# Another order of preparation for the first block of a fused attention and feed-forward kernel, with its feature sums on GpSimd

## The chip, the cores and the metric

The kernel runs on one NeuronCore of a Trainium2 chip. Five engines work side by side, each through its own instruction queue in order: TensorE (PE in the profile; its weight loads are PEld), VectorE (DVE), ScalarE (ACT), GpSimd (POOL) and SyncE (SP), which here issues all the DMAs. They wait for one another through semaphores. The metric is the device time of one execution in microseconds.

## What is computed

Attention over 4 batches, 8 heads, 576 positions and 64 features a head, and then two gated feed-forward layers over the 2304 tokens:

```python
# two attentions per head, added
q_d, k_d, v_d = (mean of 4 neighbouring positions)       # 144 positions
out_up = repeat(softmax(q_d k_d^T / 8) v_d, 4)
out_local = softmax(where(|i - j| < 4, q k^T / 8, -1e9)) v
x = (out_up + out_local) as (2304 tokens, 512)
x = silu(x @ moe_w_in) @ moe_w_out                        # 512 -> 2048 -> 512
h = x @ moe2_w_in
out = (h * sigmoid(1.702 h)) @ moe2_w_out
```

## The kernel before

**The attention part** goes through 16 units; a unit is two heads of one batch (`Unit`, number `n`). In a unit, PE makes the banded scores (`band_scores`, L1088 and L1095), then transposes the probabilities of the unit before (`group`, L1077), makes the scores of the averaged positions (`avg_scores`, L1118), and multiplies the unit before with its values (`band_product` L1147, `avg_product` L1158). DVE reduces and subtracts the maxima (L1017, L1020, L1024), sums the rows (L1030), takes the reciprocal (L1034), sums four neighbouring positions of the next unit's q and k (`sums`, L1005), and writes the unit before into `x` (L1050). ACT takes the exponentials (L944, L956), normalises (L975) and copies out of PSUM (L928, L932, L964). GpSimd sums v (L887, L895), normalises the band (L890) and makes two of the first layer's weight sums (`sum_weights`, L905 to L911). All engines run `iterations`: unit 0, units 1 to 15, and a last step 16 that only finishes unit 15.

**The feed-forward part** (`Ffn`) goes over 6 blocks of 768 tokens: 3 of the first layer, 3 of the second. It multiplies in a scheme with seven products instead of eight for a 2 by 2 division into quarters, and each factor is split into a rounded part and a rest (`xs`, `wh`, `gr`; index 0 is the rounded part, index 1 the rest), so that a product is three matmuls a tile. In `first` PE makes 8 pairs of 42 matmuls into `hid` (L309), in the order of the table `FIRST`; in `second` seven stages of 48 matmuls into `yp` (L332), in the order of `SECOND`. What the products need of a block's features are seven quarters and their sums: B11, B21, B22 as they are, T1, T3, T2, T4 as differences, made in place (`sum_x`, L256). Each is rounded by ACT (`round_x`, L241) and its rest made by DVE (`rest_x`, L245), in the order of `FILLS`.

**The order around the change** is written out by hand. For the first block this preparation is strewn into the attention units by `early`: ACT rounds the weights of batches 0 to 2 in units 3 to 5 and the features in units 6 and 8 to 13; DVE makes weight rests in units 4 to 6, feature rests in 7, 9 to 12, 14, 15 and the four sums in 8, 9, 10 and 13. ACT's `early` of unit `n` from 8 waits for `x_done` of all units up to `n-1`, and stands ahead of its normalising (L975). For the later blocks `prepare_x` does it in the stages of `second`. SP starts with the loads of q and k of two units, and issues the writing back of the first weight sums (`store_first`) only when all 16 units are written, since it stands in `ffn.sync`. PE begins with 11 matmuls on an identity (`WARM`, L1186), whose results nobody uses.

## Time and profile before

| | |
|---|---|
| median of 3 runs | 831.03 us (829.6 to 832.05) |
| profiled execution | 829.3 us, of which its span 827.4 us |
| PE busy, share of the span | 804.7 us, 97% |
| DVE / ACT / POOL busy | 655.6 / 536.1 / 176.1 us |
| attention: from the start to the first feed-forward matmul | 0 to 117.2 us |
| feed-forward: from there to the end | 117.2 to 827.4 us |

In a line of the timeline stand the start in us from the span's beginning, the time taken, the engine, the line of the code, the operation, the tile written and those read, the shapes, how many instructions are merged (x...), and in brackets how long the engine had been idle just before and what ended that. The start of one instruction and the end of the one before it on the same engine overlap by up to 0.1 us, so costs on a path are taken from start to start. A busy PE of 97% says that there is little idle time, not that the matmuls run at their fastest: 4032 of them are the feed-forward part.

### The profile page before, as it was taken

What the parts mean: (1) busy time and instruction counts of PE and PEld (TensorE: products, weight loads), DVE (VectorE), ACT (ScalarE), POOL (GpSimd) and SP (SyncE); (2) the same over time, 40 slices, a digit from 0 to 9 for tenths busy, and PEclk for the clock granted to TensorE, in tenths of its full rate; (3) what the DMA queues carried; (4) which work ended last, traced back from release to release, by engine and by line L of the source; (5) the groups of instructions that cost most, each with busy time, mean ns of one, the idle gap of its engine ahead of it and who ended that gap; (6) DMA issues with size and microseconds to landing.
All of it is one profiled execution on the core that took longest, in us unless ns stands there. A gap on an engine that the chain in (4) does not pass through costs nothing.

```text
span 827.4 us, 15637 instructions
## 1 busy us (share of the span) xinstructions
PE 804.7 (97%) x5787; PEld 776.3 (94%) x5787; DVE 655.6 (79%) x945; ACT 536.1 (65%) x864; POOL 176.1 (21%) x191
## 2 busy tenths in 40 slices
PE   7998999999999999999999999999999999999998
PEld 4776679999989999999999999999999999999997
DVE  6999959889998967798867888899756677665465
ACT  4887765567745577745578565687455777465763
POOL 6766656702025511025300000000000000000000
PEclk9999999999999999999999999999999999999999
DMA  7877748757677897768886787876987878877773
GB/s 216 241 224 208 223 147 292 255 202 258 206 259 245 270 321 257 258 203 273 263 298 237 229 264 251 268 248 229 307 270 259 268 254 265 285 255 271 256 271 125
DMA packets 98315, 205.42 MB, mean 248 GB/s; under 512 B 8416, under 2 KB 56032, under 8 KB 98240
## 3 DMA queue, kind: packets, MB, share of 16 engines
q1 hardware_dynamic: 98240, 204.42, 75.0%
q8 instruction: 47, 0.77, 0.4%
q14 instruction: 28, 0.23, 0.1%
HBM read 160.87 MB, written 43.52 MB: 247 GB/s over the span
## 4 chain that ended last, share of the span: by engine, by line
PE 79%; DVE 13%; issue 4%; ACT 2%; POOL 1%; DMA 1%; DVEq 0%; SPq 0%; POOLq 0%; ACTq 0%
PE hid L309 40%; PE yp L332 35%; DVE gr L482 2%; DVE wh L284 2%; DVE smb L1030 1%; DVE xs L245 1%; DVE x L1050 1%; PE pt L1077 1%; DVE sums L1005 1%; DVE mxb L1017 1%; DVE pband L1020 1%; PE po L1147 1%; DMA sums_in<-G 1%; ACT yt L928 1%; PE sc L1095 1%
## 5 line engine op out<-in xcount | busy, mean ns | idle before, releaser
L309 PE MATMUL hid<-xs,wh 128*128 128x384 f32 x2016 | 352.4, 334 | 3.1 <-DVE hw L462 1.8
L309 PEld LDWEIGHTS hid<-xs,wh 128*128 128x128 f32 x2016 | 349.2, 188 | 5.5 <-issue 5.2
L332 PE MATMUL yp<-gr,wh 128*128 128x384 f32 x2016 | 350.9, 334 | 1.7 <-DVE gr L482 1.7
L332 PEld LDWEIGHTS yp<-gr,wh 128*128 128x128 f32 x2016 | 349.4, 188 | 2.3 <-issue 2.3
L275 ACT ACTIVATE wh<-wr 128x1024 fp32r<-128x1024 f32 (+1 forms) x164 | 164.5, 1003 | 156.1 <-PE hid L309 122.4
L482 DVE TENSOR_TENSOR gr<-G,gr 128x768 fp32r<-128x768 f32 x144 | 138.5, 971 | 48.3 <-ACT gr L382 48.3
L382 ACT ACTIVATE gr<-G 128x768 fp32r<-128x768 f32 x144 | 121.8, 846 | 68.9 <-PE yp L332 67.6
L284 DVE TENSOR_TENSOR wh<-wr,wh 128x1024 fp32r<-128x1024 f32 x76 | 89.7, 1181 | 21.5 <-ACT wh L275 21.5
L349 ACT ACTIVATE G<-G 128x1152 f32<-128x1152 f32 x48 | 55.8, 1161 | 0.0
L457 DVE TENSOR_TENSOR hv<-p,hid 128x384 f32<-128x384 f32 x48 | 26.4, 549 | 28.4 <-PE hid L309 19.3
L472 DVE TENSOR_TENSOR G<-hv,hid 128x384 f32<-128x384 f32 x48 | 26.5, 552 | 26.5 <-PE hid L309 25.9
L245 DVE TENSOR_TENSOR xs<-x,xs 128x768 fp32r<-128x768 f32 x42 | 41.2, 981 | 5.6 <-ACT xs L241 5.6
L241 ACT ACTIVATE xs<-x 128x768 fp32r<-128x768 f32 x42 | 34.9, 832 | 10.0 <-DVE x L1050 10.0
L424 DVE TENSOR_TENSOR G<-G 128x384 f32<-128x384 f32 x48 | 29.1, 607 | 8.4 <-ACT G L349 8.4
L469 DVE TENSOR_TENSOR G<-hw,hid 128x384 f32<-128x384 f32 x48 | 26.3, 548 | 3.4 <-DMA sums_in<-G 2.3
L431 DVE TENSOR_TENSOR G<-G 128x384 f32<-128x384 f32 x48 | 28.4, 592 | 0.2
L549 POOL TENSOR_TENSOR G<-G 128x256 f32<-128x256 f32 x8 | 6.4, 806 | 103.0 <-DMA G<-in_w_in 54.5
L275 ACT ACTIVATE wh<-G 128x1024 fp32r<-128x1024 f32 (+1 forms) x16 | 15.3, 956 | 19.1 <-PE hid L309 19.1
L549 POOL TENSOR_TENSOR wt<-wt 128x256 f32<-128x256 f32 x12 | 10.4, 867 | 80.9 <-DMA wt<-in_w_out 45.9
L474 DVE TENSOR_TENSOR gr<-G,gr 128x384 fp32r<-128x384 f32 x48 | 27.4, 571 | 0.0
L462 DVE TENSOR_TENSOR hw<-hv,hid 128x384 f32<-128x384 f32 x48 | 26.3, 548 | 1.4 <-PE hid L309 0.9
L364 ACT ACTIVATE G<-hid 128x384 f32<-128x384 f32 x48 | 23.6, 492 | 5.7 <-PE hid L309 1.1
(90 smaller groups left out, 766.1 us busy)
## 6 DMA issues: line engine op xcount, KB each, us to landing
wh<-rests SPq DMA_DIRECT2D x72, 512.0 KB, 3.9
wr<-sums_out SPq DMA_DIRECT2D x48, 512.0 KB, 4.8
wr<-in_w_out SPq DMA_DIRECT2D x36, 512.0 KB, 5.2
rests<-wh SPq DMA_DIRECT2D x36, 512.0 KB, 3.4
wr<-sums_in SPq DMA_DIRECT2D x40, 384.0 KB, 4.1
wr<-in_w_in SPq DMA_DIRECT2D x40, 256.0 KB, 3.5
qk<-in_qkT SPq DMA_DIRECT2D x16, 576.0 KB, 5.4
G<-in_w_in SPq DMA_DIRECT2D x12, 512.0 KB, 6.2
```

The lines of the kernel that those rows point to most:

```text
L241: eng.activation(xs[:, 0, q], features(n, q), ACT.Copy).then_inc(self.x_hi, 1)
L245: eng.tensor_tensor(xs[:, 1, q], features(n, q), xs[:, 0, q].bitcast(F32), ALU.subtract).then_inc(self.x_lo, 1)
L275: eng.activation(wh[:, w % SLOTS, 0, 0:entries(w), :], raw(w), ACT.Copy).then_inc(w_hi, 1)
L284: eng.tensor_tensor(wh[:, w % SLOTS, 1, 0:e, :], raw(w), wh[:, w % SLOTS, 0, 0:e, :].bitcast(F32), ALU.subtract).then_inc(w_lo, 1)
L309: last = eng.matmul(hid[:, at, 0:HALF], lhsT=wh[:, w % SLOTS, part, a % 4, cc * P:(cc + 1) * P], rhs=xs[:, rest, q, cc, :], start=start an ...
L332: last = eng.matmul(yp[:, at + m, 0:HALF], lhsT=wh[:, w % SLOTS, part, p % 4, m * P:(m + 1) * P], rhs=gr[:, p, rest, :], start=start and p ...
L349: eng.activation(G[:, s % PAIRS, G12:G22 + 1, :], G[:, s % PAIRS, G12:G22 + 1, :], ACT.Silu, scale=scale).then_inc(self.gate, 1)
L382: eng.activation(gr[:, 2 * a:2 * a + 2, 0, :], G[:, 2 * a:2 * a + 2, at, :], ACT.Copy).then_inc(self.g_hi, 1)
L424: eng.tensor_tensor(G[:, p, G11, :], G[:, p, G12, :], G[:, p, G11, :], ALU.subtract).then_inc(self.t_sum, 1)
L431: eng.tensor_tensor(G[:, p, G12, :], G[:, p, G22, :], G[:, p, G12, :], ALU.subtract).then_inc(self.t_sum, 1)
L474: eng.tensor_tensor(gr[:, p, 1, :], G[:, p, G11, :], gr[:, p, 0, :].bitcast(F32), ALU.subtract).then_inc(self.b11_lo, 1)
L482: eng.tensor_tensor(gr[:, 2 * a:2 * a + 2, 1, :], G[:, 2 * a:2 * a + 2, SECOND[i][1], :], gr[:, 2 * a:2 * a + 2, 0, :].bitcast(F32), ALU.s ...
```

## The change

- `WARM` goes from 11 to 7.
- q and k get three buffers instead of two (the third is the place of `ffn.wt`), and the sums of four positions two buffers; three units are loaded at the start, and `sums` runs two units ahead: twice ahead of unit 0, and not in unit 14.
- `FILLS` has another order. `ROUNDED_W`, `ROUNDED` and `SUMMED` say in which units the first block is prepared: ACT rounds weights in 4, 6, 7 and features in 3, 5, 9, 10, 11, 13, 15; DVE makes the rests one unit later; the four sums are made by GpSimd, each in two halves of 128x384, in units 7 to 14, behind its weight sums. The wait for `x_done` is for one unit less.
- In the later blocks DVE makes each of the four sums behind another rest.
- PE makes the first three products of the first pair (18 matmuls) in step 16, ahead of the transposes of unit 15.
- ACT applies Silu to a small tile that is no longer needed, behind the normalising of unit 15.
- `store_first` for pairs 0 and 1 stands in the attention part, behind unit 15's loads.

```diff
-FILLS = (B11, T1, T3, T2, B21, B22, T4)
+FILLS = (B11, B21, T1, B22, T3, T2, T4)
...
-        def sum_x(eng, n, q):
+        def sum_x(eng, n, q, chunk=None):
...
-            eng.tensor_tensor(features(n, q), a, b, ALU.subtract).then_inc(self.x_sum, 1)
+            if chunk is None:
+                eng.tensor_tensor(features(n, q), a, b, ALU.subtract).then_inc(self.x_sum, 1)
+            else:
+                eng.tensor_tensor(features(n, q)[:, chunk], a[:, chunk], b[:, chunk], ALU.subtract).then_inc(
+                    self.x_sum if chunk else self.x_half, 1)
+                if not chunk:
+                    eng.wait_ge(self.x_half, XSUM[q])
...
-            for q in {B11: (T1, T3), T1: (T2,), B21: (T4,)}.get(FILLS[i], ()):
+            for q in {B11: (T1,), B21: (T3,), T1: (T2,), B22: (T4,)}.get(FILLS[i], ()):
...
-            def first(n, p):
+            def first(n, p, starting=False):
                 s = PAIRS * n + p
                 for i, (a, q, at, start) in enumerate(FIRST):
+                    if n == p == 0 and (i < 3) != starting:
+                        continue
...
+            if begin:
+                first(0, 0, True)
+                return
...
-            store_first(0)
-            store_first(1)
...
+    ROUNDED = (3, 5, 9, 10, 11, 13, 15)
+    ROUNDED_W = (4, 6, 7)
+    SUMMED = {7: (T1, 0), 8: (T1, 1), 9: (T3, 0), 10: (T3, 1), 11: (T2, 0), 12: (T2, 1), 13: (T4, 0), 14: (T4, 1)}
...
-    WARM = 11
+    WARM = 7
...
                 load_vwin(u)
+                load_qk(u.after().after())
                 load_vwin(u.after())
...
+            for p in range(2):
+                ffn.store_first(eng, p)
             for q in range(2):
                 eng.wait_ge(band_out, UNITS)
                 ffn.load_pair(eng, q)
...
                 sum_weights(u)
+                if u.n in SUMMED:
+                    eng.wait_ge(x_done, 1 + min(u.n - 1, 8))
+                    ffn.sum_x(eng, 0, *SUMMED[u.n])
...
+                if last:
+
+                    eng.activation(nga[:], nga[:], ACT.Silu)
...
-                    eng.wait_ge(x_done, 1 + n)
-                    ffn.round_x(eng, 0, FILLS[n - 7])
+                elif n in ROUNDED:
+                    eng.wait_ge(x_done, 1 + min(n - 1, 8))
+                    ffn.round_x(eng, 0, FILLS[ROUNDED.index(n)])
...
-                    if not last:
-                        sums(u.after())
+                    if u.n + 2 < UNITS:
+                        sums(u.after().after())
...
-                if last is not None:
+                if last is None:
+
+                    eng.wait_ge(b_sub, 2 * UNITS)
+                    eng.wait_ge(a_exp, NA * UNITS)
+                    ffn.tensor(eng, True)
+                else:
                     band_scores(u)
```

Three places of the order of instructions follow. A row has its number in the engine's queue, the line, the operation, the tile written, those read and the columns; x18 are so many in a row, and "waits" names semaphores. On DVE, before, unit 10 from the end of its maxima to the writing of unit 9 (`x<-po,oavg`); `x<-x` is a feature sum, `xs` a rest:

```order
126 L1024 TENSOR_REDUCE mxa<-hp 112x3
127 L256 TENSOR_TENSOR x<-x 128x2x384
128 L245 TENSOR_TENSOR xs<-x,xs 128x768
129 L1030 TENSOR_REDUCE smb<-pband 128x9
130 L1034 RECIPROCAL rcb<-smb 128x9
131 L1005 TENSOR_REDUCE sums<-qk 128x288
132 L1040 TENSOR_REDUCE rca<-sma 112x3
133 L1042 RECIPROCAL rca<-rca 112x3
134 L1050 TENSOR_TENSOR x<-po,oavg 128x576
```

and the same unit in the changed kernel:

```order
125 L1049 TENSOR_REDUCE mxa<-hp 112x3
126 L255 TENSOR_TENSOR xs<-x,xs 128x768
127 L1055 TENSOR_REDUCE smb<-pband 128x9
128 L1059 RECIPROCAL rcb<-smb 128x9
129 L1030 TENSOR_REDUCE sums_0<-qk 128x288
130 L1065 TENSOR_REDUCE rca<-sma 112x3
131 L1067 RECIPROCAL rca<-rca 112x3
132 L1075 TENSOR_TENSOR x<-po,oavg 128x576
```

The sum has left DVE; one rest is left in this unit. On POOL, before, two units in a row (7 and 8; `vpair` belongs to the unit that follows):

```order
64 L905 TENSOR_TENSOR G<-G 128x256 [waits w0_sum]
65 L907 TENSOR_TENSOR G<-G 128x256 [waits w0_sum]
66 L887 TENSOR_TENSOR vpair<-vn 72x512 [waits v_sum,vn_in]
67 L890 TENSOR_TENSOR pband<-pband,rcb 128x9x70 [waits b_rcp]
68 L895 TENSOR_TENSOR vavg<-vpair 72x256 [waits avg_out,v_half]
```

and two units of the changed kernel (8 and 9):

```order
66 L929 TENSOR_TENSOR G<-G 128x256 [waits w0_sum]
67 L931 TENSOR_TENSOR G<-G 128x256 [waits w0_sum]
68 L269 TENSOR_TENSOR x<-x 128x384 [waits x_sum,x_done]
69 L908 TENSOR_TENSOR vpair<-vn 72x512 [waits v_sum,vn_in,x_half]
70 L911 TENSOR_TENSOR pband<-pband,rcb 128x9x70 [waits b_rcp]
71 L916 TENSOR_TENSOR vavg<-vpair 72x256 [waits avg_out,v_half]
```

Half a feature sum now stands between the weight sums and `vpair`. On PE, before, the end of the attention part, from the scores of the averages of unit 15 on:

```order
147 L1118 MATMUL hp<-sums 48x144 x6
148 L1077 MATMUL pt<-ident,pavg 72x112 x6
149 L1147 MATMUL po<-yt,vwin 64x64 x18
150 L1158 MATMUL po<-pta,vavg 64x144 x4
151 L1077 MATMUL pt<-ident,pband 70x128 x6
152 L1077 MATMUL hp<-ident,pband 70x128 x3
153 L1077 MATMUL pt<-ident,pavg 72x112 x6
```

and in the changed kernel:

```order
143 L1143 MATMUL hp<-sums_1 48x144 x6
144 L1102 MATMUL pt<-ident,pavg 72x112 x6
145 L1172 MATMUL po<-yt,vwin 64x64 x18
146 L1183 MATMUL po<-pta,vavg 64x144 x4
147 L328 MATMUL hid<-xs,wh 128x384 x18
148 L1102 MATMUL pt<-ident,pband 70x128 x6
149 L1102 MATMUL hp<-ident,pband 70x128 x3
150 L1102 MATMUL pt<-ident,pavg 72x112 x6
```

18 matmuls of the feed-forward part now come ahead of the transposes of unit 15.

## Rows read from the trace of the kernel before

**Rows 1.** Timeline of DVE, units 4 and 5, and the start of 15.

```profile
32.72 0.88 DVE L1017 TENSOR_REDUCE mxb<-sc 128x5 f32<-128x350 f32 x2
...
35.22 1.22 DVE L284 TENSOR_TENSOR wh<-G,wh 128x1024 fp32r<-128x1024 f32 x1
...
39.49 0.87 DVE L1017 TENSOR_REDUCE mxb<-sc 128x5 f32<-128x350 f32 x2
...
41.57 1.28 DVE L284 TENSOR_TENSOR wh<-G,wh 128x768 fp32r<-128x768 f32 x1
42.77 0.81 DVE L1030 TENSOR_REDUCE smb<-pband 128x9 f32<-128x639 f32 x1
...
45.90 0.87 DVE L1017 TENSOR_REDUCE mxb<-sc 128x5 f32<-128x350 f32 x2
...
107.78 0.87 DVE L1017 TENSOR_REDUCE mxb<-sc 128x5 f32<-128x350 f32 x2
...
110.20 0.95 DVE L245 TENSOR_TENSOR xs<-x,xs 128x768 fp32r<-128x768 f32 x1
```

**Rows 2.** Timeline of PE, starts of the banded scores of units 2 and 3.

```profile
19.17 0.44 PE L1088 MATMUL sc<-band,ident 128*128 128x350 bf16 x2
...
25.13 0.44 PE L1088 MATMUL sc<-band,ident 128*128 128x350 bf16 x2
```

**Rows 3.** Timeline of all engines, from the end of unit 10 into unit 11.

```profile
79.61 0.74 DVE L1050 TENSOR_TENSOR x<-po,oavg 128x576 f32<-128x576 f32 x1
...
80.38 0.84 ACT L241 ACTIVATE xs<-x 128x768 fp32r<-128x768 f32 x1 [1.86 <-DVE x L1050]
...
83.16 0.72 ACT L944 ACTIVATE pband<-pband 128x630 f32<-128x630 f32 x1
...
83.92 0.82 DVE L1030 TENSOR_REDUCE smb<-pband 128x9 f32<-128x639 f32 x1 [0.31 <-ACT pband L944]
```

**Rows 4.** Timeline of POOL, units 5 and 6, and a weight sum later.

```profile
40.75 1.28 POOL L887 TENSOR_TENSOR vpair<-vn 72x512 f32<-72x512 f32 x1
43.91 1.24 POOL L890 TENSOR_TENSOR pband<-pband,rcb 128x630 f32<-128x630 f32 x1 [1.88 <-DVE rcb L1034]
45.11 0.73 POOL L895 TENSOR_TENSOR vavg<-vpair 72x256 f32<-72x256 f32 x1
...
47.29 1.28 POOL L887 TENSOR_TENSOR vpair<-vn 72x512 f32<-72x512 f32 x1
...
134.07 1.79 POOL L554 TENSOR_TENSOR wt<-wt 128x256 f32<-128x256 f32 x1
```

**Rows 5.** Timeline of the first units.

```profile
8.08 0.88 DVE L1017 TENSOR_REDUCE mxb<-sc 128x5 f32<-128x350 f32 x2 [2.09 <-PE sc L1095]
...
13.13 1.43 PE L1077 MATMUL pt<-ident,pband 128*70 128x128 f32 x6 [1.68 <-POOL pband L890]
...
20.69 0.85 PE L1077 MATMUL pt<-ident,pband 128*70 128x128 f32 x6
```

**Rows 6.** Windows: stretch, length, each engine's busy time, PE clock, DMA share, GB/s.

```profile
14.00:15.00 1.00, 1.00 (x6) 0.66 (x4) 0.71 (x2) 1.00 (x3) 1.00 (x2) 0.50 0.29 115
```

**Rows 7.** DMAs issued up to 3 us: operation, count, KB, us to landing.

```profile
qk<-in_qkT SPq DMA_DIRECT2D x2, 576.0 KB, 4.4
```

**Rows 8.** Timeline of the end of the attention part.

```profile
113.60 0.82 PE L1077 MATMUL pt<-ident,pband 128*70 128x128 f32 x6 [1.50 <-POOL pband L890]
...
117.23 6.53 PE L309 MATMUL hid<-xs,wh 128*128 128x384 f32 x36
...
118.64 0.49 ACT L357 ACTIVATE p<-hid 128x384 f32<-128x384 f32 x1 [1.02 <-PE hid L309]
...
122.79 1.28 ACT L364 ACT_TABLE_LOAD   x1 [0.18 <-PE hid L309]
```

**Rows 9.** Timeline of PE alone, the feed-forward part.

```profile
124.25 52.27 PE L309 MATMUL hid<-xs,wh 128*128 128x384 f32 x300 [0.49 <-DVE G L469]
...
228.16 8.56 PE L332 MATMUL yp<-gr,wh 128*128 128x384 f32 x48 [1.72 <-DVE gr L482]
```

More of the change, by code:

```diff
@@ L99, in __init__ @@
         self.w_hi, self.w_lo = sem("w_hi"), sem("w_lo")
-        self.x_sum, self.x_hi, self.x_lo = (sem(n) for n in ("x_sum", "x_hi", "x_lo"))
+        self.x_half, self.x_sum, self.x_hi, self.x_lo = (sem(n) for n in ("x_half", "x_sum", "x_hi", "x_lo"))
         self.product, self.pair = sem("product"), sem("pair")
@@ L122, in first_operands, with store_sums, store_first @@
         return self.G[:, p].rearrange("p s n -> p (s n)")[:, a * 256:b * 256].rearrange("p (a n) -> p a n", n=256)
+    def store_sums(self, eng, src, to_three, to_one, done):
+        eng.dma_start(to_three, src[:, 0:3, :]).then_inc(done, DMA_INC)
+        eng.dma_start(to_one, src[:, S4, :]).then_inc(done, DMA_INC)
+    def store_first(self, eng, p):
+        to = self.wi[0, p]
+        eng.wait_ge(self.w0_sum, 4 * (p + 1))
+        self.store_sums(eng, self.first_operands(p, 0, 7), to[:, 0:3, :], to[:, 3, :], self.w0_out[p])
     def tile(self, q):
@@ L608, in store_rest @@
                     self.rest_out[w % SLOTS], DMA_INC)
-            def store_sums(src, to_three, to_one, done):
-                eng.dma_start(to_three, src[:, 0:3, :]).then_inc(done, DMA_INC)
-                eng.dma_start(to_one, src[:, S4, :]).then_inc(done, DMA_INC)
             def store_pair(q):
@@ L620, in store_pair @@
                     to = self.wo[q // 16].rearrange("a p n c -> p n a c")[:, p]
-                store_sums(self.tile(q), to[:, 0:3, :], to[:, 3, :], done)
+                self.store_sums(eng, self.tile(q), to[:, 0:3, :], to[:, 3, :], done)
             def load_pair(q):
@@ L656, in batch @@
                         if n == 0 and p + 2 < PAIRS:
-                            store_first(p + 2)
+                            self.store_first(eng, p + 2)
                         if 1 <= p < 7:
@@ L742, in build @@
             vavg = sb("vavg", [P, 2, 2 * D])
-            qk = sb("qk", [P, 2, 2, S])
-            sums4 = sb("sums4", [P, 2, SD])
+            two = sb("qk", [P, 2, 2, S])
+            qk = [two[:, 0], two[:, 1], ffn.wt[:].rearrange("p a n -> p (a n)")[:, 0:2 * S].rearrange(
+                "p (i s) -> p i s", i=2)]
+            sums4 = [sb(f"sums4_{i}", [P, 2, SD]) for i in range(2)]
             pband = [sb(f"pband{i}", [P, NT, WIN + 1]) for i in range(2)]
@@ L770, in build @@
         vn_in = sem("vn_in")
-        qk_in = [sem(f"qk_in{i}") for i in range(2)]
+        qk_in = [sem(f"qk_in{i}") for i in range(3)]
         qk_sum = sem("qk_sum")
@@ L823, in body @@
                     load_vn(u.after())
-                if u.n + 2 < UNITS:
+                if u.n + 3 < UNITS:
                     if first:
@@ L831, in body @@
                         eng.wait_ge(qk_sum, u.n + 1)
-                    load_qk(u.after().after())
+                    load_qk(u.after().after().after())
                 if u.n + 1 < UNITS:
@@ L1002, in sums @@
             def sums(u):
-                eng.wait_ge(avg_sc, u.n)
-                eng.wait_ge(qk_in[u.odd], DMA_INC * (u.half + 1))
-                eng.tensor_reduce(sums4[:], qk[:, u.odd, :, :].rearrange(
+                if u.n > 1:
+                    eng.wait_ge(avg_sc, u.n - 1)
+                eng.wait_ge(qk_in[u.n % 3], DMA_INC * (u.n // 3 + 1))
+                eng.tensor_reduce(sums4[u.odd][:], qk[u.n % 3].rearrange(
                     "p i (s r) -> p i s r", r=FACTOR), AX.X, ALU.add).then_inc(qk_sum, 1)
@@ L1070, in _, with start @@
             eng.sem_inc(x_done, 1)
-            iterations(eng, sums, body)
+            def start(u):
+                sums(u)
+                sums(u.after())
+            iterations(eng, start, body)
             ffn.vector(eng)
@@ L1083, in band_scores @@
             def band_scores(u):
-                eng.wait_ge(qk_in[u.odd], DMA_INC * (u.half + 1))
+                eng.wait_ge(qk_in[u.n % 3], DMA_INC * (u.n // 3 + 1))
                 eng.wait_ge(b_sub, 2 * u.n)
@@ L1095, in head_scores @@
                     return eng.matmul(sc[half, bank, (t - a) * WIN:(t - a + 1) * WIN],
-                                      lhsT=qk[rows, u.odd, 0, t * QT:(t + 1) * QT],
-                                      rhs=qk[rows, u.odd, 1, starts[t]:starts[t] + WIN],
+                                      lhsT=qk[u.n % 3][rows, 0, t * QT:(t + 1) * QT],
+                                      rhs=qk[u.n % 3][rows, 1, starts[t]:starts[t] + WIN],
                                       start=False, stop=t in (LEFT - 1, NT - 1), skip_group_check=True)
@@ L1118, in avg_scores @@
                         last = eng.matmul(sa[h * QT:h * QT + AQ, c * SD:(c + 1) * SD],
-                                          lhsT=sums4[rows, 0, c * AQ:(c + 1) * AQ], rhs=sums4[rows, 1, :],
+                                          lhsT=sums4[u.odd][rows, 0, c * AQ:(c + 1) * AQ], rhs=sums4[u.odd][rows, 1, :],
                                           start=True, stop=True)
```

28 lines of the change are left out of this document (8 added, 20 removed).

## The prediction

> **What bounds the kernel now.** I read first the timeline of PE alone. From 124.25 us to the end it runs almost without a gap, 300 matmuls in 52.27 us or 0.174 us each [rows 9], and its largest gap there is 1.72 us. The change leaves those 4032 matmuls as they are, so time can only come from before 124.25 us, or from that gap.
>
> Then I went through the units by the starts of the first maximum (L1017) on DVE. From unit 4 to unit 15 they go from 32.72 to 107.78 us, eleven units in 75.06 us, or 6.82 us a unit [rows 1]. PE alone needs 5.96 us for one, from one unit's scores to the next [rows 2]. So PE is not the bound of the middle units. Two others are. Unit 5 shows the first: 39.49 to 45.90 is 6.41 us, of which 41.57 to 42.77, 1.20 us, is the strewn-in weight rest. Without it DVE needs **5.21 us** [rows 1]. The end of unit 10 shows the second: ACT stood idle 1.86 us until DVE had written `x` (L1050), rounded, normalised, copied, and came to the band's exponential only at 83.16; DVE had to wait for it (0.31 us) before its row sum at 83.92 [rows 3]. The reader is to see a loop there: `x` on DVE, rounding and normalising on ACT, row sum on DVE.
>
> **The change, part by part.**
>
> *DVE's middle units.* A unit lasts 5.21 us plus what is strewn in. A clean rest of 128x768 costs 0.87 (0.95 less the overlap of 0.08 with its successor), of 128x1024 1.14 [rows 1]. In unit 5 the 768 columns cost 1.20, 0.33 more; POOL's `vpair` ran from 40.75 to 42.03 and the rest began in it at 41.57 [rows 1, 4]. I charge these 0.33 us in every unit with a rest from 5 on, for the halves put on POOL keep it busy at that place. Bounds for this charge: 0, and a whole POOL instruction of about 1 us. I take 0.33, since POOL goes through the same instructions up to there.
>
> The loop over ACT goes: its rounding now waits for a unit that was written a unit ago, so it falls where ACT stood idle. What remains is DVE's own path to the exponential. From `x` to the end of the subtraction are 0.66 + 0.79 + 0.79 us (0.74 [rows 3] and twice 0.87 [rows 1], the subtraction being as long as the maximum, each less the overlap) and 0.1 for the handing over, 2.35; the exponential and the handing back are 83.16 to 83.92, 0.76 [rows 3]; from the row sum to the next unit's maximum 42.77 to 45.90, 3.13, and `x` lies 0.66 before that [rows 1]. A unit without a rest thus lasts 2.35 + 0.76 + 2.47 = 5.6 us, not 5.21.
>
> Could PE or POOL hold these? POOL's normalising starts 1.99 us before the next maximum and takes 1.24 [rows 1, 4], then PE needs its 5.96: at least 1.24 - 1.99 + 5.96 = 5.2 us from one maximum to the next; no hold. POOL goes from L890 to the end of `vpair` in 47.29 + 1.28 - 43.91 = 4.66 us [rows 4]. A half of 384 columns lies between the 256 (0.73) and 512 columns (1.28) there: 1.0 us. 5.66 a unit: level with the shortest units, covered in the others. The sum is needed a unit later by ACT, about 1.8 us after POOL has it. With that cover gone POOL would set the pace (below).
>
> The eleven units:
> - 4: 5.21 + 0.87 + 0.42 (the stop of this unit beyond 5.21 + 1.14 within its 6.77) = 6.50
> - 5 and 8, with 1024 columns: 5.21 + 1.14 + 0.33 = 6.68, twice 13.36
> - 6, 7, 10, 11, 12: 5.21 + 0.87 + 0.33 = 6.41, five times 32.05
> - 9, 13: 5.60, and 14, which has a rest but no `sums` (about 1.2 us): also 5.60; together 16.80
>
> In all 68.71 against 75.06: **6.35 us** less. The sums that leave DVE and the ACT wait are both in this figure; neither alone would give it.
>
> *The start.* PE's seven warm-up matmuls end 1.7 us sooner (four of 0.43 us), but DVE now has two `sums` ahead of its first maximum. The two loads land after 4.4 us in the middle, the first at 3.8 by the wait it ends, so the second about 5.0 us after its issue at 1.2: 6.2 us [rows 7]. The second `sums` then runs to about 7.5 and the maximum starts at 7.6 rather than 8.08 [rows 5]: 0.5 us. What follows is the same chain. Bounds: nothing (a late landing) and 0.9 (PE's scores end near 7.1). The third load pushes the first weights back by some 1.7 us; they were needed by POOL at 13.6, and POOL has that much idle time before its next normalising.
>
> The six transposes at 13.13 took 1.43 us, the same at 20.69 only 0.85 [rows 5]: the granted clock is 0.50 behind the first of them, that is 1.2 GHz [rows 6], after PE had stood for 1.68 us. From the one to the other are 7.56 us where 5.96 would do. I leave this 1.6 us as it is, since the same stops precede it, and count it as a bound on both sides.
>
> *The end.* All is 0.5 + 6.35 = 6.85 us earlier, so PE is done with unit 14 at 113.60 - 1.50 - 6.85 = 105.25 [rows 8], and unit 15's last exponential is there at about 105.3. PE makes its 18 products to 108.4 (18 x 0.174 = 3.1), where it stood idle 1.5 us before; then unit 15's transposes and products, 113.60 to 117.23, 3.63: 112.0. The fourth product ends at 113.1. The fifth waits for ACT's copy of the first, 118.64 + 0.45 - 117.23 = 1.86 after PE's last attention matmul [rows 8]: 113.9, 0.8 us of idle PE. Two DVE additions of 0.55 us let the sixth start at 115.0, and the 42nd matmul ends at 117.1. Before, it ended at 124.25 + 6 x 0.174 = 125.3 [rows 9]. Gain up to there: **8.2 us**, 6.85 brought along and 1.35 of the end itself. PE's stop of 0.49 us before 124.25 [rows 9], on the addition into the tile whose sums are being written back (L469), is gone, since these DMAs are now issued some 8 us before; what is late next is ACT's copy.
>
> The table load (1.28 us at 122.79) [rows 8] moves to ACT behind the normalising of unit 15, at about 106.8, and ends at 108.1 with the small Silu at 108.3; PE's transposes, which feed ACT's next copy, end near 108.9. Cost nothing; cover 0.6 us. The row shows 0.18 us of idle time before the load and none behind it. The Trainium skill (ScalarE: Activation LUTs, What ACT_TABLE_LOAD costs) adds a drain of 1.38 us to the load; by that the end would be some 0.8 us later, and the row here does not show such a drain.
>
> *The later blocks.* DVE's total up to the end of each block's fifth stage is the same; one sum leaves stage 0 and one leaves stage 4 for stages 1 to 3. In that block's stages DVE has no idle time between its instructions, so PE's stop of 1.72 us at 228.16 [rows 9] stays. Cost 0; bounds 1.7 us gained, 1 us (one sum) lost.
>
> **Sum.** 829.3 - 8.2 = 821.1 us for the profiled execution. The median shown is 831.03, 1.7 above that execution, so I forecast **822.8 us**.
>
> **Rivals.**
> - *Port.* Each of the rests in units 8, 10, 11, 12 waits for a whole POOL instruction instead of 0.33 us: 4 x 0.65 = 2.6 us, 825.4. For it: POOL is now inside an instruction at that moment in every unit. Against: what is left of it in unit 5's case was 0.46 us.
> - *Cold PE.* With fewer warm-up matmuls the lower clock lasts a unit longer: 1.6 to 6 us more, 826 in the middle. For it: PE fell to it once, after stops as the new start has them. Against: from unit 1 on PE is busy.
> - *Upside.* The cold stretch or the stop at 228.16 goes: 821.1.
> - *Slower: POOL becomes the bound.* A weight sum of 256 columns took 1.79 us at 134.07 instead of 0.73, a factor 2.45 [rows 4]. If a half grows with it to 2.4 us, a unit on POOL is 4.66 + 2.4 = 7.06 us, and eight of them give back all of the middle: 8 x (7.06 - 6.85) = 1.7 us slower there, 829 or 830 with the other gains. It decides from halves of 2.5 us; for clearly slower, 834, they must take 2.9, a factor 3. Against: in all units the rows of POOL stay at 0.73. The Trainium skill (SBUF — State Buffer, SBUF: two separate sides) says that DVE with two SBUF inputs and GpSimd lock a shared pair of ports for a whole instruction, the other blocking. The rest that began in `vpair` agrees in kind; it bears on this rival and on *Port*.
>
> **How the numbers follow.** Forecast 0.63; Port 0.12; Cold PE 0.10; Upside 0.10; POOL the bound 0.05, of it 0.03 for clearly slower. The range reaches down for the start's bound, the uncharged collisions and the cold stretch, not all at once, to 820.0, and up over both small rivals to 827.5. About 0.3%, 2.5 us, is what a measurement of this kernel can tell from no change. Faster by more than that: 0.90; within it 0.06; slower 0.04.
>
> **What would show it.** First maximum at 7.6 us; that of unit 15 near 100.9; units 9 and 13 near 5.6 us apart from the next; ACT's waits for `x` at the rounding gone; POOL's halves near 1.0 us; 18 matmuls from 105.3; the last attention matmul near 112.0; no wait of DVE for a DMA at 117. I am wrong if units stay at 6.8 us, or if PE's stops after 125 us grow.

## The result and the profile after

| | before | after |
|---|---|---|
| median of 22 runs each | 829.59 us (828.27 to 833.36) | 828.46 us (824.52 to 830.75) |
| ratio, 95% interval | | 0.9974 (0.9962 to 0.9987) |
| profiled execution, of it the span | 829.3, 827.4 us | 825.26, 823.5 us |
| PE / DVE / ACT / POOL busy | 804.7 / 655.6 / 536.1 / 176.1 us | 802.8 / 649.8 / 537.0 / 189.9 us |

The changed kernel is 0.26% faster, some 2 us, where 8.2 us were forecast. 822.8 us was wrong, and the time lies above the range too. The forecast started from 831.03 us, a median of 3 runs; by the 22 runs above it the kernel before takes 829.59, so the forecast time lies 1.4 us nearer to the measured one than it would from that start, by luck. Two repeats beside other kernels gave 0.9961 (0.9947 to 0.9975) and 0.9972 (0.9954 to 0.999). Medians and ranges in this document are of all runs, and the ratios leave out a slow run, of which there was a single one (837.64 us, below).

The timeline of DVE after, to be held against [rows 1, 5]: the first maxima of units 0, 4, 9, 10 and 15, the second `sums` and the one in unit 9.

```profile
6.39 1.35 DVE L1030 TENSOR_REDUCE sums<-qk 128x288 f32<-128x1152 f32 x1 [0.56 <-DMA qk<-in_qkT]
7.66 0.87 DVE L1042 TENSOR_REDUCE mxb<-sc 128x5 f32<-128x350 f32 x2
...
33.21 0.88 DVE L1042 TENSOR_REDUCE mxb<-sc 128x5 f32<-128x350 f32 x2
...
65.84 0.87 DVE L1042 TENSOR_REDUCE mxb<-sc 128x5 f32<-128x350 f32 x2
...
71.03 1.35 DVE L1030 TENSOR_REDUCE sums<-wt 128x288 f32<-128x1152 f32 x1 [1.67 <-DMA wt<-in_qkT]
...
73.24 0.87 DVE L1042 TENSOR_REDUCE mxb<-sc 128x5 f32<-128x350 f32 x2
...
104.35 0.88 DVE L1042 TENSOR_REDUCE mxb<-sc 128x5 f32<-128x350 f32 x2
```

The start is as forecast, 7.66 us. But the eleven units take 104.35 - 33.21 = 71.14 us, not 68.71. Unit 9, which begins at 65.84, shows why: it should be a short one, 5.6, and takes 7.40, with a wait of 1.67 us for the load of q and k into the third buffer (`wt`). Before, no wait of DVE for such a load stood in the trace from 8 us on. Two smaller ones (0.34 and 0.42 us, in units 11 and 13) bring the waits in these units to 2.43 us, as much as the units are longer than forecast. That the two figures are equal is partly chance, since single units differ from the forecast by up to 0.4 us either way besides (unit 10: 6.14 instead of 6.41, unit 12: 6.77).

The waits of engines for DMAs from 8 to 125 us, after (engine, what, line; us in total, times, longest). Left out is POOL's wait of 5.9 us for a pair of the second weights, behind the attention part (before: 4.7):

```profile
...
POOL vpair L908 <- DMA vn<-in_v: 2.3, 2, 1.8
DVE sums L1030 <- DMA wt<-in_qkT: 2.1, 2, 1.7
POOL G L934 <- DMA G<-in_w_in: 1.7, 2, 1.0
DVE sums L1030 <- DMA qk<-in_qkT: 1.1, 3, 0.4
```

This profiled execution was one of the quick ones (825.26 against the median of 828.46). In the profile of the second repeat (span 826.8 us) the same view has much more in it:

```profile
POOL G L934 <- DMA G<-in_w_in: 8.7, 4, 3.4
...
DVE sums L1030 <- DMA wt<-in_qkT: 4.7, 4, 2.0
DVE sums L1030 <- DMA qk<-in_qkT: 4.5, 4, 1.8
POOL vpair L908 <- DMA vn<-in_v: 4.2, 3, 2.3
```

and its units 4 to 14 take 75.52 us, as long as before the change:

```profile
32.78 0.87 DVE L1042 TENSOR_REDUCE mxb<-sc 128x5 f32<-128x350 f32 x2
...
108.30 0.88 DVE L1042 TENSOR_REDUCE mxb<-sc 128x5 f32<-128x350 f32 x2
```

In such an execution all of the middle's 6.35 us is gone, with 9.2 us of waits of DVE and 12.9 of POOL for loads, and unit 4 begins no earlier than before either (32.78 against 32.72 us). What is left is the end. The first repeat lies between the two: its units take 105.33 - 32.73 = 72.60 us.

The rate of the transfers: windows of 32 to 101 us, of before and then of after (length, busy times, clock, share of the DMA engines' time, GB/s):

```profile
32.00:101.00 69.00, 62.00 (x1111) 47.88 (x1111) 66.40 (x125) 54.83 (x179) 45.85 (x52) 1.00 0.76 222
```

```profile
32.00:101.00 69.00, 64.04 (x1160) 50.33 (x1161) 64.40 (x128) 58.89 (x186) 57.16 (x62) 1.00 0.78 223
```

A unit loads 576 KB of q and k, 288 of v for POOL, 315 of v in windows, and half of a 512 KB weight pair: 1435 KB or 1.47 MB. At 6.82 us a unit that is 215 GB/s; at the forecast mean of 6.25 us it would be 235 GB/s. The last two of the eleven units load no q and k, though. Units 4 to 12 load 9 x 1179 KB and four weight pairs, 12.96 MB: 211 GB/s over their 61.48 us before, 225 over the 68.71 - 2 x 5.60 = 57.51 us forecast. So 7% more was asked of the transfers. The rate measured stayed where it was.

These 222 or 223 GB/s are no ceiling of the transfers: over its whole span the changed kernel moved 249 GB/s in the same execution, in some of the 40 slices over 300 (the page's own line):

```profile
DMA packets 98314, 205.41 MB, mean 249 GB/s; under 512 B 8416, under 2 KB 56032, under 8 KB 98240
```

In the feed-forward part, 130 to 800 us, it is 259 GB/s at a DMA share of 0.78, the same share as here. So the rate in the units is not a measured limit.

The end of the attention part on PE, for [rows 8, 9], with ACT's table load from its own timeline:

```profile
109.11 3.36 PE L328 MATMUL hid<-xs,wh 128*128 128x384 f32 x18 [0.27 <-issue]
112.31 0.82 PE L1102 MATMUL pt<-ident,pband 128*70 128x128 f32 x6
...
117.79 7.45 PE L328 MATMUL hid<-xs,wh 128*128 128x384 f32 x40 [0.54 <-ACT p L379]
```

```profile
110.86 1.28 ACT L996 ACT_TABLE_LOAD   x1
```

18 products in 3.2 us (3.1 forecast), unit 15's transposes and products from 112.31 to 115.94, 3.63 as forecast, the fifth product 1.85 us behind them (1.86). Only the beginning of the 18 products lies farther from unit 15's maximum than forecast, 4.76 us instead of 4.32. The table load costs nothing: PE goes on.

### The profile page after: what moved, and what is told of

Same layout as the page of the kernel before. It is cut to its first block, busy times and chain, and to the rows that moved or that the text cites. A ratio compares the mean times of both kernels' runs of the same rounds, so it can differ in the third digit from the quotient of the medians.

```text
span 823.5 us, 15638 instructions
## 1 busy us (share of the span) xinstructions
PE 802.8 (97%) x5783; PEld 776.3 (94%) x5783; DVE 649.8 (79%) x941; ACT 537.0 (65%) x865; POOL 189.9 (23%) x199
## 4 chain that ended last, share of the span: by engine, by line
PE 79%; DVE 10%; POOL 4%; issue 4%; DMA 2%; ACT 1%; SPq 0%; DVEq 0%; POOLq 0%; ACTq 0%
PE hid L328 41%; PE yp L351 32%; DVE gr L504 3%; DVE wh L300 3%; PE pt L1102 2%; POOL vpair L908 1%; DVE xs L255 1%; PE po L1172 1%; POOL pband L911 1%; DMA vn<-in_v 1%; PE hp L1143 1%; DVE G L462 1%; PE sc L1120 1%; DMA qk<-in_qkT 1%; POOL x L269 1%
## 5 line engine op out<-in xcount | busy, mean ns | idle before, releaser
L494 DVE TENSOR_TENSOR G<-hv,hid 128x384 f32<-128x384 f32 x48 | 26.4, 551 | 25.6 <-PE hid L328 25.3
L446 DVE TENSOR_TENSOR G<-G 128x384 f32<-128x384 f32 x48 | 27.9, 582 | 8.8 <-ACT G L371 8.8
L453 DVE TENSOR_TENSOR G<-G 128x384 f32<-128x384 f32 x48 | 27.8, 579 | 0.2
L499 DVE TENSOR_TENSOR G<-hv,hid 128x384 f32<-128x384 f32 x48 | 26.4, 551 | 0.6
```

Of the source, the lines that this page charges most:

```text
L446: eng.tensor_tensor(G[:, p, G11, :], G[:, p, G12, :], G[:, p, G11, :], ALU.subtract).then_inc(self.t_sum, 1)
L453: eng.tensor_tensor(G[:, p, G12, :], G[:, p, G22, :], G[:, p, G12, :], ALU.subtract).then_inc(self.t_sum, 1)
```

## The experiments

Each kernel ran beside the kernel before on the same chip, and the ratio is to that one. The changed kernel ran beside them only in the first and the last group; its three ratios are 0.9974, 0.9961 and 0.9972, 0.9969 in the mean.

**The changed kernel again.**

> The changed kernel unchanged, another execution. Theory A (loads of q and k land too late for the sums two units ahead): its profile again shows DVE waiting for qk or its third buffer before L1030 in units 9, 11 or 13, in all 1.5 to 5 us, the place moving from one execution to the next; its times spread over 5 us or more. Rival B (only TensorE's low-clock stretch near 12 to 19 us differs between executions): those waits stay at 2.4 us and the time follows the length of that stretch alone.

826.73 us, 0.9961 (0.9947 to 0.9975). Its profile has the granted clock at 1.00 throughout and still a span of 824.4 us, with 7.6 us of waits of DVE for q and k.

**`sums` one unit ahead, with three buffers.**

```diff
-                    if u.n + 2 < UNITS:
-                        sums(u.after().after())
+                    if not last:
+                        sums(u.after())
```

> The changed kernel with the three q/k buffers, but the sums of four positions made one unit ahead as before. Theory A: the waits of DVE for q and k after unit 1 vanish (they need each load a whole unit later), unit 9 falls from 7.4 to 5.6 us, and the time is 2 to 4 us under the changed kernel's (about 825). Rival B: no change within 0.5 us, or 0.4 us slower by the start.

825.99 us, 0.9957 (0.9942 to 0.9972), the same as the changed kernel beside it, where 2 to 4 us less were expected. DVE's waits for DMAs are gone, and POOL waits instead, ahead of its normalising, which PE waits for:

```profile
POOL G L934 <- DMA G<-in_w_in: 8.4, 6, 2.5
POOL vpair L908 <- DMA vn<-in_v: 6.7, 8, 2.1
```

The wait moved, the time did not. That DVE needed the third buffer too early is not the cause.

**Eleven warm-up matmuls** (`WARM = 11`).

> The changed kernel with 11 warm-up matmuls. Rival B: the low-clock stretch shrinks from 6 to about 3.5 us, which gives 1 to 2 us back. Theory A: the first maximum moves from 7.66 to about 8.1 us and the time stays within 0.5 us of the changed kernel.

826.17 us, 0.9953 (0.994 to 0.9965), against 0.9961 for the changed kernel beside it: the four matmuls are worth nothing that can be measured.

**POOL's rows of v left out.** The load of 288 KB is issued for unit 0 alone; the kernel leaves out the later units' averaged values.

```diff
                     eng.wait_ge(v_half, u.n + 1)
-                    load_vn(u.after())
...
-                eng.wait_ge(vn_in, DMA_INC * (u.n + 1))
+                eng.wait_ge(vn_in, DMA_INC)
```

> The changed kernel without the loads of v for GpSimd after unit 0 (it sums unit 0's v for every unit; a fifth of a unit's DMA bytes left out, its output is not the reference's). Theory A with bandwidth as the cause: the waits for q and k go to under 0.5 us in all and the time falls by 2 to 4 us. Theory A with the late issue as the cause (SP issues the load behind GpSimd's v sum): the load is issued at the same moment and waits shrink by less than half. Rival B: no change.

822.26 us, 0.9905 (0.9892 to 0.9918): 7.9 us less than before. With a fifth of the bytes gone, the eleven units and the moment of unit 15 come out as forecast:

```profile
32.16 0.88 DVE L1041 TENSOR_REDUCE mxb<-sc 128x5 f32<-128x350 f32 x2
...
100.74 0.88 DVE L1041 TENSOR_REDUCE mxb<-sc 128x5 f32<-128x350 f32 x2 [0.25 <-PE sc L1119]
```

```profile
32.00:101.00 69.00, 66.08 (x1207) 52.14 (x1203) 66.37 (x131) 60.98 (x197) 59.99 (x62) 1.00 0.58 176
```

68.58 us for the eleven units (forecast 68.71), unit 15's maximum at 100.74 (100.9). The DMA engines' share fell from 0.78 to 0.58. Two theories are left: the transfers' rate, or POOL's own wait for these rows (one buffer, and SP's load of q and k behind it).

**Queries and keys issued first.** SP issued a unit's q and k behind the wait for `vpair`, and POOL's halves push `vpair` back. In the profile after, POOL's `vpair` of unit 8 ended at 63.91 and SP issued the load that DVE waited for at 71.03 only then, though its buffer had been free since about 59.3:

```profile
60.70 1.00 POOL L269 TENSOR_TENSOR x<-x 128x384 f32<-128x384 f32 x1
61.78 2.13 POOL L908 TENSOR_TENSOR vpair<-vn 72x512 f32<-72x512 f32 x1
```

```profile
63.94 0.30 SPq L822 DMA_DIRECT2D vn<-in_v  x1
64.34 1.44 SPq L819 DMA_DIRECT2D wt<-in_qkT  x1
```

```diff
-                if u.n + 1 < UNITS:
-                    eng.wait_ge(v_half, u.n + 1)
-                    load_vn(u.after())
...
                     load_qk(u.after().after().after())
+                if u.n + 1 < UNITS:
+                    eng.wait_ge(v_half, u.n + 1)
+                    load_vn(u.after())
```

> The changed kernel, with SyncE issuing a unit's queries and keys ahead of the feature-major rows for GpSimd, so that they no longer stand behind the wait for GpSimd's vpair (in the changed kernel's trace the load of 64.34 us followed that wait by one issue, 5 us after the scores of unit 8 had freed the buffer, and landed at 71.03, where VectorE had waited 1.67 us). Theory 1, late issue: VectorE's waits for a DMA in units 4 to 14 go (2.4 us in that trace), the time falls to 822.5 to 824. Theory 2, the transfers' own rate: with the same bytes a unit something else lands late instead, GpSimd waits for its rows or for the first weights and passes it on, the time stays at 825.5 to 827. Low-clock stretch as in the changed kernel, 0 to 6 us.

> The version with queries and keys issued first, once more. If order alone is worth something, 1 to 3 us less than the changed kernel beside it (824 to 826); if not, the same within 1 us.

824.92 us, 0.9929 (0.9901 to 0.9956), and the second time 824.35, 0.9934 (0.9913 to 0.9955): 2.4 us less than the changed kernel beside the second, 3.2 and 3.3 us by the ratios. The intervals of the second and of the changed kernel (0.9954 to 0.999) just touch. From 8 us on DVE waits for no DMA any more, and POOL waits for its rows, 17.8 us in the first profile. So the order in SP's queue is part of it, and not all.

**Two buffers for POOL's rows as well**, on top of q and k first.

```diff
+            vns = [sb("vn", [HP, 2, FACTOR * 2 * D])[:], ffn.yt[:]...[0:HP, 0:2 * FACTOR * 2 * D]...]
...
-                if u.n + 1 < UNITS:
+                if u.n + 2 < UNITS:
                     eng.wait_ge(v_half, u.n + 1)
-                    load_vn(u.after())
+                    load_vn(u.after().after())
```

> qkfirst, and a second buffer for the rows of GpSimd (in the tile that holds a weight pair later), so that they are loaded a unit earlier. The same bytes, but every load except the windows and the first weights now has a unit of slack. Theory 1, late issue or too little slack: nearly all waits of VectorE and GpSimd for a DMA go and the time comes to that without these loads, 822 to 823.5. Theory 2, the transfers' rate: 1.4 MB in 6.2 us a unit are 225 GB/s beside the 224 GB/s measured over the changed kernel's whole span, so there is nothing to win by order; waits appear elsewhere and the time stays within 1 us of qkfirst's.

826.92 us over ten runs, which scatter widely: nine from 821.37 to 828.95, the tenth 837.64. The ratio is 0.9933 (0.9906 to 0.996), no better than the order alone. Its timeline shows what a load goes through. SP issued this one as soon as the buffer was free, and DVE waited for it all the same:

```profile
58.23 0.38 SPq L820 DMA_DIRECT2D wt<-in_qkT  x1
```

```profile
69.60 1.35 DVE L1032 TENSOR_REDUCE sums<-wt 128x288 f32<-128x1152 f32 x1 [1.18 <-DMA wt<-in_qkT]
```

11.4 us from issue to landing, where a load of the same size took 4.4 us in [rows 7]. In the median of 20 to 105 us the loads of q and k take 10.1 us into `qk` and 7.9 into `wt`, against 5.5 and 5.3 in the changed kernel's profile. The loads issued earlier landed later after their issue, and the time did not fall.

**No idle PE at the start.** 13 matmuls into a free accumulator, 7 ahead of unit 1's banded scores and 6 behind them.

```diff
+                if u.n == 1:
+                    for i in range(6):
+                        eng.matmul(po[:, 512 * (i % 2):512 * (i % 2) + 512], lhsT=ident16[:], ...)
...
+                if u.n == 0:
+                    for i in range(7):
+                        eng.matmul(po[:, 512 * (i % 2):512 * (i % 2) + 512], lhsT=ident16[:], ...)
```

> The changed kernel, with 6 matmuls of 512 columns into a free accumulator behind unit 0's averaged scores and 7 ahead of unit 0's transposes, so that TensorE does not stand idle between units 0 and 1. Theory 1, the low clock is part of what is missing: the granted clock stays at 1.00 from 4 us on in every execution, the start gets 0.9 us shorter than in the changed kernel's profile and the median falls by 0.8 to 2 us. Theory 2: what is gained there is waited away for the loads in the units behind it; median 826 to 827, and the sum of the DMA waits in the attention part is longer by what the start is shorter.

827.62 us, 0.9967 (0.995 to 0.9983). The clock was 1.00 all through its profile, and nothing came of it: DVE waited 9.4 us for loads, POOL 15 us. The low clock is not what keeps the time up: where it is absent, the time is the same.

**The end alone, on the kernel before.** The 18 early products, the small Silu, `store_first` in the attention part; of the diff above nothing else.

> The kernel before, with only the end part of the change: 18 products of the first block ahead of unit 15's transposes, the small Silu behind the last normalising, and the stores of the first weight sums issued by SyncE ahead of the pair loads. No change of the units. By the prediction's sum 1.35 us less than before (0.9984), and nothing more. Rival: the end's gain hangs on units that come 7 us earlier (the sums' stores leave in time either way); then 0 to 0.5 us.

829.48 us, 0.998 (0.9967 to 0.9992), 1.7 us less by the ratio (0.7 to 2.7); 1.35 forecast. The end's term fits.

The profile, of the slowest of the twelve runs (832.17 us), shows something else. Its units and loads are those of the kernel before, and here too loads of q and k came late: PE waited 1.6 us for one, DVE 1.6 us for one, units 4 to 14 took 111.52 - 33.29 = 78.23 us, and the granted clock was 0.83 from 60 to 80 us.

**Bytes, taken away elsewhere and added.** Three kernels: the window loads of v (315 KB) left out from unit 2 on, and with them the later units' values; POOL's rows left out of the kernel before; a further 288 KB a unit into an unused tile, for which SP first waits until the one before has landed. The main lines of the first and the last edit (the second is that of the run without POOL's rows, on the kernel before):

```diff
                         eng.wait_ge(band_out, u.n)
-                        load_vwin(u.after())
```

```diff
                     load_vn(u.after())
+                    load_extra(u.after())
```

> The changed kernel, with the windows of v (315 KB a unit) loaded for the first two units alone; TensorE takes these for every unit. GpSimd's own rows (288 KB) and all waits of SyncE stay as they are. It leaves out part of the computation: the values of the later units. Theory 1, the transfers' rate is the bound: whichever 300 KB a unit are left out, the time is that of the run without GpSimd's rows, 822 to 823.5, and VectorE's waits for a DMA in units 4 to 14 go. Theory 2, only GpSimd's wait for its rows, with one buffer, was the trouble: nothing of it goes here, 825.5 to 827.

> The kernel before, with GpSimd's rows (288 KB a unit) loaded for the first unit alone (it leaves out part of the computation: the averaged values of the later units). Theory 1: with units of 6.8 us the loads had just time enough, so here the bytes are worth little, 0 to 1.5 us (0.998 to 1.0), against 7.9 us in the changed kernel: the bound by the transfers is new. Rival: the transfers bound the kernel before in the same degree; then 4 us or more.

> The changed kernel, with a further load of 288 KB a unit into a tile nobody reads (units 1 to 15). Theory 1, the transfers' rate: 288 KB at 225 GB/s are 1.28 us a unit, 19 us over 15 units, less what slack there is; 835 to 846, with longer waits of VectorE and GpSimd for DMAs. Theory 2, rate to spare and only late issue: the load lies in the gaps, 826 to 830.

822.61 us, 0.9919 (0.9903 to 0.9935) without the windows: it matters little which 300 KB go. 829.01, 0.9994 (0.9984 to 1.0005) for the kernel before without POOL's rows: there they cost nothing that can be measured. 844.64, 1.0176 (1.0153 to 1.02) with 288 KB more: against the changed kernel's mean ratio of 0.9969 that is 2.1% or 17 us for 15 x 288 KB = 4.4 MB, 1 us for each 260 KB. At the 226 GB/s measured, 4.4 MB take 19.6 us, so most of it lies on the path. The windows of the last:

```profile
32.00:101.00 69.00, 55.86 (x982) 42.60 (x981) 54.02 (x105) 49.90 (x161) 48.87 (x51) 1.00 0.85 226
```

Every engine is busy for less of the time, and the rate is 226 GB/s, hardly more than the 222 and 223 of the two kernels above.

**The first weights a unit earlier too**, on two buffers for POOL's rows.

```diff
-                if u.odd and u.n + 1 < UNITS:
-                    eng.wait_ge(ffn.w0_sum, 2 * u.n)
+                if not u.odd and u.half + 1 < UNITS // 2:
                     ffn.first_raw(eng, u.half + 1)
```

> The version of before with two buffers for GpSimd's rows and the queries and keys issued first, and now the first weights a unit earlier too (in the even units, without waiting for the sums before them). The same bytes, each load with a unit or more of slack. Theory 1, the mean rate of 230 GB/s a unit just does for 6.2 us a unit and only uneven arrival costs: GpSimd's waits for the first weights (2.47 and 1.96 us there) go, the median comes to 822.5 to 824.5. Theory 2, the rate itself: a load of queries and keys lands later than before (12.5 us there at the worst), VectorE waits for it, and the median stays at 825 to 827.

827.85 us (820.08 to 830.89), 0.9962 (0.9937 to 0.9986), outside both expectations. The profiled execution is the second best, 821.47 us, with unit 15's maximum where the prediction had it, all bytes moved, and no wait of DVE for a load from 8 us on:

```profile
100.53 0.88 DVE L1043 TENSOR_REDUCE mxb<-sc 128x5 f32<-128x350 f32 x2 [0.25 <-PE sc L1121]
```

Eight of the twelve runs were at 827.5 or more. In the profile units 4 to 12 take 58.28 us at 222 GB/s, no more than the 226 GB/s of the kernel before over its own units 4 to 12. So neither the bytes nor the rate rule out the forecast time. The slower runs have no profile, and whether their loads came late is not shown. For the changed kernel it is: its three profiles have 3.2, 7.6 and 9.2 us of waits of DVE for loads, and 71.14, 72.60 and 75.52 us for units 4 to 14, with the same program. What makes the loads later in one execution than in another stays open.

**Bytes moved out of the shortened units.** Five instead of six later weight loads up to unit 12, the last two in units 14 and 15, where no q and k are loaded any more; their sums behind unit 15 on POOL. First with q and k first and two buffers for POOL's rows, then with q and k first and one buffer.

```diff
+    LOADED = (1, 4, 7, 10, 12, 14, 15)
+    ADDED = (0, 3, 6, 9, 12, 14)
...
-                if u.odd and u.n + 1 < UNITS:
-                    eng.wait_ge(ffn.w0_sum, 2 * u.n)
-                    ffn.first_raw(eng, u.half + 1)
+                if u.n in LOADED:
+                    ffn.first_raw(eng, LOADED.index(u.n) + 1)
...
+            for p in (6, 7):
+                sum_half(p, 0)
+                sum_half(p, 1)
```

> Two buffers for GpSimd's rows, queries and keys issued first, and the first weights spread thinner: five of their seven later loads in units 1 to 12 instead of six in units 1 to 11 with sums for each in two units, the last two loads in units 14 and 15, behind the last load of queries and keys, and their sums behind unit 15 on GpSimd, where it stood idle 5.9 us. Per unit about 85 KB less of 1.4 MB up to unit 12. Theory 1, the transfers' rate: a third of what 288 KB gave, 2 to 3 us less than the changed kernel, 823 to 825, with fewer waits for DMAs. Rival: the scatter from execution to execution is the transfers' own and the median stays at 826 to 828; or GpSimd's late sums delay the second layer's pairs and TensorE stops longer after 125 us.

> As the one before, but with one buffer for GpSimd's rows. If bytes count, as that one, 823 to 825; if a unit of slack for the rows counts as well, 1 us more, with GpSimd's waits for its rows of 1 to 2 us as in the version with queries and keys first.

> The changed kernel itself, as the measure for the others on this chip: 826 to 828.5.

821.22 us (820.76 to 826.04), 0.9908 (0.9884 to 0.9932), and 822.28 us (820.95 to 824.4), 0.9916 (0.9895 to 0.9936), against 826.78 for the changed kernel beside them, 0.9972 (0.9954 to 0.999). Both compute everything, and the first is the fastest complete kernel of the study: 8 us below the kernel before, 5.5 below the changed one, and below the 823 to 825 expected. This is three edits together. Against q and k first alone, beside it, the moved bytes of the second version are worth 2.1 us (0.9916 against 0.9934), with intervals that overlap. They also take weight sums from POOL in four of the units, which no run separates; the run without POOL's rows reached the same unit times with these sums in place. The first version's units 4 to 14 take 68.22 us:

```profile
33.70 0.88 DVE L1054 TENSOR_REDUCE mxb<-sc 128x5 f32<-128x350 f32 x2
...
101.92 0.88 DVE L1054 TENSOR_REDUCE mxb<-sc 128x5 f32<-128x350 f32 x2 [0.25 <-PE sc L1132]
```

```profile
32.00:101.00 69.00, 66.47 (x1221) 52.26 (x1219) 66.34 (x133) 61.47 (x199) 55.76 (x57) 1.00 0.83 210
```

It moved 210 GB/s in this window, the changed kernel 223. The number alone does not tell the two cases apart: the second repeat of the changed kernel, with units of 75.52 us in all, had 214.

## Why the prediction was wrong

**The step that failed** is the bound of the middle, -6.35 us, from which the loads are missing. The working bounded the units by DVE (5.21), by the path over ACT (5.6), by PE (5.96 from scores to scores) and by POOL (5.66), and never by the transfers. By the count of bytes, units 4 to 12 need 225 GB/s at the forecast length instead of 211. In the trace of before a load of q and k took 6.1 us to land in the median, nearly a unit, and it could have been asked what becomes of that. It showed no wait of DVE for q and k; that was room at 6.8 us a unit and not at 6.25. The loads came late instead, and DVE and POOL waited for them: 2.43 us of the middle in the profile after, all 6.35 in that of the second repeat. The runs that leave out 288 or 315 KB a unit come out at 822.26 and 822.61 us, 7.9 and 6.7 us below the kernel before instead of the 8.2 forecast; the one that adds 288 KB loses 17 us; and the kernel before gains at most 0.2% without 288 KB. In the ordinary execution the bound is thus new, made by the shorter units. It is a bound by loads that land late, and which property of the transfers sets the moment stays open, since the same kernel moves 259 GB/s in its feed-forward part, and a run with the forecast units needed 222. In single executions late loads also reach the old units, as the profile of the kernel with the end alone shows.

**A second step was missing, in SP's queue.** The halves went to POOL ahead of `vpair` of the next unit; SP waits for that `vpair` with the load of q and k queued behind. The prediction named POOL's 5.66 us a unit and not SP behind it. It is worth 2.4 to 3.3 us by the runs with q and k first. The two steps are not independent terms: with the bytes gone and the order as it was, the time is lower still.

**Where the sum was right by luck.** In the run without POOL's rows, units 9 to 14 take 100.74 - 64.80 = 35.94 us, and 36.03 were forecast. But the rests of units 10, 11 and 12 took 0.95, 1.05 and 1.14 us there, so the collision cost 0 to 0.2 us and not 0.33. As far as the trace shows, PE held these units: from 64 to 101 us it is busy for 36.02 of 37.00 us, and six times its 5.96 [rows 2] is 35.76. POOL is next to it, busy for 36.40 us, of which 2.8 are what four stretched `vpair` (below) take beyond 1.28. The prediction held PE's 5.96 against a single unit, where it found room down to 5.2 us, and not against the row of units 9 to 14. So with the loads in time, the next gain in these units would have to come from PE and POOL.

**Point by point.**
- First maximum at 7.6: 7.66. The third load was charged to the first weights only. POOL's wait for `vn` at 8 us is not new (1.84 us against 1.92), its wait for the first weights at 14 us is: 1.03 us here, 0.42 to 2.77 in the profiles of the variants, none in the kernel before.
- Cold stretch left as it is, bounds 1.6 us either way: in the profile after, the clock is at 0.50 for some 6.8 us instead of 3.4, and the stretch from one group of transposes to the next takes 21.18 - 12.71 = 8.47 us against 7.56, 0.9 us more, within the bound. In the two other profiles of the same kernel the low clock is absent and 3.4 us long. Rival *Cold PE* is right about that one execution and does not explain the median: without any low clock the time is the same.

```profile
12.71 1.46 PE L1102 MATMUL pt<-ident,pband 128*70 128x128 f32 x6 [1.68 <-POOL pband L911]
...
21.18 0.85 PE L1102 MATMUL pt<-ident,pband 128*70 128x128 f32 x6
```

- Middle, -6.35: -3.92 in the quick profiled execution, -2.46 in the first repeat, nothing in the second; by the same count -6.48 in the run without POOL's rows, -5.30 without the windows and -6.84 with the bytes moved. What the prediction says of DVE and ACT was right in the main. ACT's wait of 1.86 us for `x` [rows 3] is gone: the rounding at 77.55 follows directly on the copy before it.

```profile
77.55 0.85 ACT L251 ACTIVATE xs<-x 128x768 fp32r<-128x768 f32 x1
```

- Collisions of DVE and POOL, 0.33 us in each unit with a rest: the charge holds up to unit 8 in the run without POOL's rows (units of 6.41 to 6.68 us) and is too high in 10 to 12 (6.42, 6.20 and 6.27). And POOL pays as well. In the profile after, `vpair` took 2.13 us at 61.78 beside DVE's rest, and a half 1.97 at 81.30, where 1.28 and 1.00 are usual. `vpair` is stretched to 1.86 us or more in three units of that profile, in six and five of the two repeats, and in none before. *Port* charged more of it to DVE; it fell on POOL, and through SP on the loads.
- *POOL the bound*: halves take 1.00 us as forecast, 1.97 at the most. It did not decide, but little was missing, as said above. (Its sum has 6.85, the whole gain, where the length of a unit, 6.82, belongs: 1.9 us instead of 1.7.)
- End, -1.35: the kernel before with the end alone gained 1.7 us (0.7 to 2.7), and the intervals of the trace are those forecast but for the 0.44 us ahead of the 18 products. The table load leaves no idle time here either: it takes 1.28 us, and the small Silu begins at 112.15, 0.01 us behind it.
- Later blocks, 0: the stop of [rows 9] is 1.44 us now instead of 1.72; one of 0.84 us is new, two around 600 us have become one of 0.79. In sum PE's stops behind 125 us grew by 0.66 us (4.22 to 4.88), which the prediction had named as a sign of being wrong.

```profile
223.78 8.56 PE L351 MATMUL yp<-gr,wh 128*128 128x384 f32 x48 [1.44 <-DVE gr L504]
...
576.60 8.58 PE L351 MATMUL yp<-gr,wh 128*128 128x384 f32 x48 [0.84 <-DVE gr L504]
```

Against the sum for the profiled execution, 821.1, it took 825.26: 0.99 us are there by unit 4 (low clock), 2.43 come in units 4 to 14 (loads), 0.4 between unit 15's maximum and the 18 products, and the rest, 0.3, behind them. The median lies 3.2 us above that execution again. As far as the three profiles show, it was one in which the loads kept up rather well.

## What to carry to other kernels

When a change shortens a loop, divide the bytes that its passes load by the new length, compare it with the rate now, and ask of each load how much of a pass it takes to land. That there is no wait for a DMA at the old length says nothing about the new one. The rate of now is no ceiling (7% more was asked for here, and one version had the units forecast at 222 GB/s), but a need above it is a warning to be priced in the range. Here an independent load issued ahead of a wait (2.4 to 3.3 us) and bytes moved out of the shortened stretch (some 2 us more, not clear of noise) paid, and more buffers alone did not. And follow a step that is moved into an engine's queue on to the queues that wait for that engine, SP's loads among them.

## What the runs showed of the hardware

- A load takes longer to land with others about: 576 KB of q and k landed in 4.4 us [rows 7] and, issued as soon as the buffer was free in the version with more buffers, in 11.4 us. The median of these loads from issue to landing, 20 to 105 us, was 6.1 us in the kernel before, 3.8 us there without POOL's rows.
- The share of time in which the DMA engines are busy says little of the rate: 0.76 with 222 GB/s in the kernel before, 0.83 with 210 in the fastest version (both 32 to 101 us), and in the changed kernel 0.78 with 223 there and 0.78 with 259 from 130 to 800 us.
- The same program waits for its loads for different times in different executions: 3.2, 7.6 and 9.2 us of DVE in three profiles of the changed kernel. The scatter is not only the clock's: one kernel had 820.08 and 828.05 us at a mean granted clock of 1.00 in both. The kernel before scatters as well, by 5 to 8 us in its groups of runs.
- DVE and POOL held each other up in turn. In the profile after, POOL's half ran from 60.70 to 61.70, DVE's rest of 128x1024 from 61.41 to 62.79 (1.38 us where 1.22 is usual), and `vpair` from 61.78 to 63.91 (2.13 instead of 1.28).
- The granted clock of 0.50 lasted 6.8, 0 and 3.4 us in the three profiles of the changed kernel. PE had stood for 1.68 us ahead of unit 0's transposes in all three. Filling the stops changed the time by less than could be measured.
